# Attention scores as 64x64 tiles in the four quarters of the array, with two PSUM banks fewer for turned rows and probabilities

## The reference, cut to what matters

```python
# q, k, v: (4, 8, 576, 64);  window 128
scores = q @ k.T / 8                       # per batch and head
mask = (rel >= 0) & (rel < 128)            # rel = query position - key position
scores = where(mask, scores - slope[head] * abs(rel), -1e9)
attn = softmax(scores);  x = attn @ v      # x: 2304 rows of 512
x = moe(x, w_gate, w1, w2)                 # each token to one of 8 experts, 288 tokens each, by sorted logits
h = x @ w_in;  out = (h * sigmoid(h)) @ w_out
```

## Time and profile before

| | |
|---|---|
| time, 3 runs | 860.46, 860.61 (median), 862.47 us |
| the profiled execution: its time, its span | 861.91 us, 860.2 us |
| busy share of the span: PE, PEld, DVE, ACT, POOL | 96%, 90%, 57%, 38%, 36% |
| scores in attention, 192 columns | 224 matmul records |
| DMA queues, share of 16 engines | 28.7% for the main queue over the span |

### The profile page before, as it was taken

One profiled execution on the slowest core, in us unless ns is written; L12 is line 12 of the kernel. 1 busy time (PEld: TensorE's weight loads), 2 busy tenths in 40 slices (PEclk: granted clock), 3 DMA queues, 4 the chain that ended last, 5 costly groups with the idle time before them and its releaser, 6 DMA issues.

```text
span 860.2 us, 17129 instructions
## 1 busy us (share of the span) xinstructions
PE 827.4 (96%) x6459; PEld 773.0 (90%) x6459; DVE 494.5 (57%) x1590; ACT 330.3 (38%) x767; POOL 306.7 (36%) x336
## 2 busy tenths in 40 slices
PE   5999999937999999999999999999999999999997
PEld 5999999926988998999899888998998899899996
DVE  7778787665855666475655443756556566542111
ACT  3655566513323432433343224333432433343221
POOL 1443333502435323523433235234332623433223
PEclk9999999957999999999999999999999999999999
DMA  9887888305104303230430040404301240431000
GB/s 148 179 169 160 174 165 172 103 14 171 54 1 126 111 13 98 67 86 2 126 106 18 1 126 13 123 2 126 99 26 45 83 123 2 127 88 36 1 1 37
DMA packets 154626, 71.39 MB, mean 83 GB/s; under 512 B 98992, under 2 KB 140976, under 8 KB 154544
## 3 DMA queue, kind: packets, MB, share of 16 engines
q1 hardware_dynamic: 149200, 60.56, 28.7%
q0 software_dynamic: 2976, 9.44, 3.6%
q10 hardware_dynamic: 2368, 0.30, 0.3%
HBM read 60.83 MB, written 9.44 MB: 82 GB/s over the span
## 4 chain that ended last, share of the span: by engine, by line
PE 74%; DVE 3%; POOL 1%; issue 1%; DMA 1%; ACT 0%; SPq 0%; POOLq 0%; DVEq 0%
PE hp L1127 12%; PE hp L1128 11%; PE hp L1129 11%; PE acc L1212 8%; PE acc L1214 8%; PE acc L1213 8%; PE acc L1127 4%; PE acc L1129 4%; PE acc L1128 4%; PE rt L1079 2%; DVE test L1379 1%; DMA wa_raw<-in_moe_w_dram 1%; PE rt L1094 0%; DVE test L1375 0%; PE acc L1121 0%
## 5 line engine op out<-in xcount | busy, mean ns | idle before, releaser
L1055 POOL TENSOR_TENSOR h_l<-h_raw,h_h 128x256 fp32r<-128x256 f32 (+1 forms) x128 | 115.5, 903 | 265.5 <-ACT h_h L1336 265.3
L1605 DVE TENSOR_TENSOR h_raw<-hp,gate 128x256 f32<-128x256 f32 (+1 forms) x128 | 58.5, 457 | 179.9 <-ACT gate L1328 179.0
L1127 PE MATMUL hp<-xy_h,res_h 128*128 128x256 f32 (+1 forms) x512 | 154.0, 301 | 0.0
L1128 PE MATMUL hp<-xy_l,res_h 128*128 128x256 f32 (+1 forms) x512 | 151.4, 296 | 0.0
L1129 PE MATMUL hp<-xy_h,res_l 128*128 128x256 f32 (+1 forms) x512 | 151.2, 295 | 0.0
L1043 POOL TENSOR_TENSOR wb_l<-wb_raw,wb_h 128x512 fp32r<-128x512 f32 x64 | 86.6, 1354 | 125.6 <-ACT wb_h L1272 125.5
L1328 ACT ACTIVATE gate<-hp 128x256 f32<-128x256 f32 (+1 forms) x128 | 52.6, 411 | 195.4 <-PE hp L1129 193.7
L1212 PE MATMUL acc<-res_h,h_h 128*128 128x512 f32 x288 | 116.7, 405 | 0.0
L1214 PE MATMUL acc<-res_h,h_l 128*128 128x512 f32 x288 | 113.5, 394 | 0.0
L1213 PE MATMUL acc<-res_l,h_h 128*128 128x512 f32 x288 | 113.5, 394 | 0.0
L1127 PEld LDWEIGHTS hp<-xy_h,res_h 128*128 128x128 f32 x512 | 96.5, 188 | 3.6
(11 more groups left out here) (216 smaller groups left out, 1684.3 us busy)
## 6 DMA issues: line engine op xcount, KB each, us to landing
wa_raw<-in_moe_w_dram SPq DMA_DIRECT2D x64, 256.0 KB, 3.3
wb_raw<-in_moe_w_dram SPq DMA_DIRECT2D x64, 256.0 KB, 3.0
k_rows<-in_k_dram SPq DMA_DIRECT2D x64, 72.0 KB, 3.7
q_rows<-in_q_dram SPq DMA_DIRECT2D x60, 72.0 KB, 2.7
v_rows<-in_v_dram SPq DMA_DIRECT2D x32, 128.0 KB, 2.5
stage<-in_moe_w_in_dram SPq DMA_DIRECT2D x8, 512.0 KB, 4.6
x_rows<-x_rows_sb SPq DMA_DIRECT2D x16, 256.0 KB, 4.2
stage<-in_moe_w_out_dram SPq DMA_DIRECT2D x8, 512.0 KB, 4.3
```

The costliest lines, as they stand in the source:

```text
L1055: pool.tensor_tensor(h_l[:, cols], h_raw[:, cols], h_h[:, cols].bitcast(FP32), ALU.subtract).then_inc(g_low, 1)
L1127: nc.tensor.matmul(out_, weights_h, cols_h, start=start, stop=False)
L1128: nc.tensor.matmul(out_, weights_h, cols_l, start=False, stop=False)
L1605: nc.vector.tensor_tensor(h_raw[:, h_cols(s, f)], hp[(A_NO[s, f] - 1) % 2][:, 0:width], gate[:, 0:width], ALU.mult).then_inc(g_done, 1)
```

## The change

Scores are computed without the zero blocks. For each unit and each head there is one matmul with 64 rows and 64 columns of weights, placed with `tile_position` in one quarter of the array. Head 0 uses rows 0 to 63, head 1 rows 64 to 127. An even unit's heads go to columns 0 and 64, an odd unit's to 64 and 0, so that two units with two heads name each quarter once. Even and odd units have banks of their own (`s_even`, `s_odd`, two each). In odd units head 1 therefore stands on partitions 0 to 63: `bias` has a form for each parity, and `turn_probs` writes their two heads in reverse. `t_ps` and `m_ps` have one bank each. `turn_probs(s)` now waits for `copy_probs(s - 1)`. The end of the turned output rows comes a slot later than the main part, `gate_logits` two slots later than `turn_x_main`, and `add_logits` a slot later than before.

```diff
 def unit_col(u):
     return {0: KEYS, 1: KEYS + U, UNITS - 1: 0}.get(u, KEYS * (u % 2))
+def bank_col(u):
+    return KEYS if u == 0 else 0
...
-        qT = [sb(f"qT{i}", [P, UNITS, P]) for i in range(2)]
+        qT = [sb(f"qT{i}", [P, S]) for i in range(2)]
...
-        s_ps, t_ps, o_ps, m_ps = pb("s_ps"), pb("t_ps"), pb("o_ps"), pb("m_ps")
+        s_ps = [pb("s_even"), pb("s_odd")]
+        t_ps, o_ps, m_ps = pb("t_ps", 1)[0], pb("o_ps"), pb("m_ps", 1)[0]
+        x_banks = [(m_ps, m_ps)] * (NG - 1) + [(s_ps[0][1], s_ps[1][1])]
...
             def turn_x_main(g):
-                if g >= 1:
-                    pe.wait_ge(x_taken, g)
+                if 1 <= g < NG - 1:
+                    pe.wait_ge(lg_added, g)
...
             def turn_x_end(g):
-                if g >= 1:
-                    pe.wait_ge(lg_added, g)
+                pe.wait_ge(x_taken, g + 1)
...
             def scores(s):
                     k0, kw = unit_keys(u)
-                    c = unit_col(u)
-                    last = nc.tensor.matmul(s_ps[s % 2][:, c:c + kw], qT[g % 2][:, u, :], kT[g % 2][:, k0:k0 + kw],
-                                            start=True, stop=True)
+                    c = bank_col(u)
+                    for h in range(2):
+                        at, side = slice(U * h, U * (h + 1)), h ^ (u % 2)
+                        to = slice(U * side, U * (side + 1))
+                        last = nc.tensor.matmul(s_ps[u % 2][s % 2][to, c:c + kw], qT[g % 2][at, U * u:U * (u + 1)],
+                                                kT[g % 2][at, k0:k0 + kw], start=True, stop=True,
+                                                tile_position=(U * h, U * side))
                 last.then_inc(s_done, 1)
...
             def turn_probs(s):
                 pe.wait_ge(exp_done, UNITS_TO[s + 1])
-                if s >= 2:
-                    pe.wait_ge(pT_ready, s - 1)
+                if s >= 1:
+                    pe.wait_ge(pT_ready, s)
...
                 if kind == 2 and g >= 1:
                     turn_x_main(g - 1)
+                if kind == 3 and g >= 1:
                     turn_x_end(g - 1)
-                if kind == 3 and g >= 1:
-                    gate_logits(g - 1, slice(0, TB))
+                if kind == 0 and g >= 2:
+                    gate_logits(g - 2, slice(0, TB))
             turn_x_main(NG - 1)
             weighted_values(NS - 1)
-            pe.wait_ge(lg_added, NG - 1)
             gate_logits(NG - 1, slice(0, main_tiles(NG - 1)))
...
                 if kind == 3 and g >= 1:
                     copy_x(g - 1)
-                    copy_x_end(g - 1)
+                if kind == 0 and g >= 2:
+                    copy_x_end(g - 2)
                 if s + 1 < NS:
                     exponentials(s + 1)
                 copy_probs(s)
...
-            def turn_q(g, h):
+            def turn_q(g):
...
-                nc.vector.transpose(qT[g % 2][at, :, at],
-                                    q_rows[g % RING_IN][at].rearrange("p n d -> p (n d)").rearrange("p (u m) -> p u m", m=U)
-                                    ).then_inc(q_turned, 1)
+                nc.vector.transpose(qT[g % 2][:], q_rows[g % RING_IN][:].rearrange("p n d -> p (n d)")).then_inc(q_turned, 1)
...
+            def make_bias(pair):
+
+                nc.vector.scalar_tensor_tensor(bias[:, pair], steep[:], 2.0 ** (-16.0 * pair / H),
+                                               masked[:, None, :].to_broadcast([P, 2, KEYS]), ALU.mult, ALU.add
+                                               ).then_inc(bias_ready, 1)
```

More of the change, by code:

```diff
@@ L454, in turn_probs @@
                     region, parity = divmod(n, 2)
-                    to = t_ps[s % 2][:, 2 * P * region:2 * P * (region + 1)].rearrange("p (h u m) -> p h u m", h=2, u=2)
-                    last = nc.tensor.transpose(to[:, :, parity, :], from_, ident[:])
+                    to = t_ps[:, 2 * P * region:2 * P * (region + 1)].rearrange("p (h u m) -> p h u m", h=2, u=2)
+                    to = to[:, ::-1 if parity and (s % 4 or region) else 1, parity, :]
+                    last = nc.tensor.transpose(to, from_, ident[:])
                 last.then_inc(t_done, 1)
@@ L548, in copy_probs @@
                 w = slice(2 * P if s == 0 else 0, 2 * P if s == NS - 1 else 4 * P)
-                nc.scalar.activation(pT[s % 2][:, w], t_ps[s % 2][:, w], ACT.Copy).then_inc(pT_ready, 1)
+                nc.scalar.activation(pT[s % 2][:, w], t_ps[:, w], ACT.Copy).then_inc(pT_ready, 1)
             load_squares(act, q_rows, q, 0, q_loaded[0])
@@ L675, in _ @@
             nc.vector.memset(p_first[:, U:P], 0.0).then_inc(pads_ready, 1)
[L676 to L681, removed]
+            for side in range(2):
+                dve.wait_ge(pool_seq, 1)
+                at = slice(U * side, U * (side + 1))
+                for parity in range(2):
+                    nc.vector.tensor_scalar(steep[at, parity, :], rel[at, :], -float(U) * side,
+                                            -(D ** 0.5) * 2.0 ** (-8.0 * ((side ^ parity) + 1) / H), ALU.add, ALU.mult
+                                            ).then_inc(steep_ready, 1)
             nc.vector.tensor_scalar(rel[U:P, :], rel[U:P, :], -float(U), None, ALU.add).then_inc(rel_ready, 1)
@@ L691, in _ @@
             dve.wait_ge(dve_seq, 3)
[L692 to L695, removed]
+            dve.wait_ge(steep_ready, 4)
+            def make_bias(pair):
+                nc.vector.scalar_tensor_tensor(bias[:, pair], steep[:], 2.0 ** (-16.0 * pair / H),
+                                               masked[:, None, :].to_broadcast([P, 2, KEYS]), ALU.mult, ALU.add
+                                               ).then_inc(bias_ready, 1)
+            make_bias(0)
             turn_k(0)
-            turn_q(0, 0)
-            turn_q(0, 1)
-            dve.wait_ge(bias_ready, PAIRS)
+            turn_q(0)
+            dve.wait_ge(bias_ready, 1)
             bias_and_max(0)
@@ L702, in _ @@
             bias_and_max(1)
-            turn_q(1, 0)
+            turn_q(1)
             for s in range(NS):
                 g, kind = divmod(s, 4)
-                if kind == 0 and g >= 2:
+                if kind == 1 and g >= 2:
                     add_logits(g - 2)
                 if s + 2 < NS:
+                    if kind == 2 and 1 <= g + 1 < PAIRS:
+                        dve.wait_ge(bias_ready, g + 2)
                     bias_and_max(s + 2)
+                if kind == 0 and g + 1 < PAIRS:
+                    make_bias(g + 1)
                 if s >= 1:
@@ L714, in _ @@
                 if kind == 3 and g + 2 < NG:
-                    turn_q(g + 2, 0)
-                if kind == 0 and g + 1 < NG:
-                    turn_q(g + 1, 1)
+                    turn_q(g + 2)
                 if kind >= 1 and g >= PAIRS + 1 and g % PAIRS == 1:
                     rank_batch(g // PAIRS - 1, kind - 1)
+            add_logits(NG - 2)
             normalise(NS - 1)
```

35 lines of the change are left out of this document (15 added, 20 removed).

## The result

The changed kernel took 867.47 us (median of 4 runs, 866.88 to 868.99) against 860.6 us (4 runs, 860.46 to 862.47): a ratio of 1.0075, 95% interval 1.0062 to 1.0087, slower by 6.9 us. The forecast was 888 us. The sign came out as forecast and the size did not. The experiments show that the sign was luck: the scores themselves became faster, and these four executions were slower for another reason. Of twelve more executions of the same kernel, half were faster than the kernel before (experiment 9).

A forecast was written before the change was run, and what follows sets the result against it. PE was taken to bound steady attention, so only its queue counted. +27.0 us for scores and +0.5 for the end, on the median 860.6, gave 888 us; range 845 to 908, likeliest case 876 to 900.

The forecast's parts named there:

- (a): Scores' arithmetic: quarters start in order, eight records filling five periods, 0.815 us a plain slot, 0.16 us more than before.
- The weight loads, as a bound: Lower bound of a slot's scores: eight weight loads following each other at 0.054 us, 0.43 us.
- (b): Change between full array and quarters, twice a slot: 0.33 us a slot, the upper end, taken as a choice.
- The sum of the scores: Plain slot's scores, arithmetic plus mode changes: 1.145 us, 0.44 more than 0.70; +27.0 us over 16 pairs.
- overlap in full, and border in full: Rival for slot scores: 0.43 + 0.33 = 0.76 us against 0.70, no change within a few us, 858 to 867; chance 0.10.
- starts in order, borders free: Rival for slot scores: ordered starts cost 8.6 us, mode changes nothing; 869 us, spread 864 to 874; chance 0.17.
- (c): `turn_q`, one transpose of 128 partitions for two of 64: DVE saves 0.77 us a pair, time gains nothing.
- (d): Probabilities' one bank: `turn_probs(s)` waits for `copy_probs(s - 1)`, with 0.74 us of cover; taken as nothing.
- (e): Output rows in one bank, chain stretched one step a slot: nothing, at worst 0.3 us a pair (5 us).
- (f): End of attention: last pair but one's gate matmuls a slot later, one wait gone; within 1 us, +0.5 in the sum.
- (g): Start: first scores a microsecond or two earlier, gain given back at pair 1's queries and slot 2's maximum; nothing.
- a third way: Way the forecast could be wrong, to the slow side: granted clock below 1.00 in steady attention; no size given.

The follow-up runs named there:

- experiment 9: Changed kernel without an edit, twelve more executions: six from 858.27 to 859.14 us, six from 866.64 to 884.57 us; ratio 1.0014.
- experiment 12: Changed kernel with five filling transposes, each slot's score matmuls issued twice from slot 8 on: 878.14 us in one execution.
- experiment 7: Changed kernel with five filling transposes, odd units' heads not in reverse, so four matmuls share two quarters: 875.13 us in one execution.
- experiment 8: Kernel before, full-width scores, with only the change's single banks and later output rows, gate and addition: 861.72 us against 861.53, 1.0007.
- experiment 1: Kernel before with 40 transposes of the identity ahead of its first scores: 861.19 us against 861.52, 0.9996.
- experiment 4: Changed kernel with five transposes of the identity in PE's pause at 11 us: 857.79 us against 861.52, 0.9955.
- experiment 5: Changed kernel with three matmuls in one quarter filling the pause at 11 us: 867.52 to 875.72 us, 1.0106.
- experiment 11: Changed kernel with five transposes of the identity in slot 1, where PE does not wait: 859.29 us against 861.69, 0.9967.
- experiment 13: Changed kernel with three matmuls in one quarter added in slot 1: 868.69 to 886.03 us, median 874.3, 1.0143.
- experiment 14: Changed kernel with five transposes in the pause at 11 us, timed again: 858.49 us against 861.45, 0.9958.
- experiment 6: Changed kernel with 16 transposes of the identity in slot 4: 860.69 us against 861.53, 1.0008.
- experiment 10: Changed kernel with 38 transposes ahead of the scores and 18 in the pause behind the first turned probabilities: 858.32 us against 861.69, 0.9956.
- experiment 2: Changed kernel with 38 transposes of the identity ahead of its first scores: 867.18, 867.46, 875.04 and 884.53 us.
- experiment 3: Kernel before, slot 3's scores made to wait for slot 2's maxima, so PE pauses: 863.02 us against 861.52, 1.0017.

## Why the prediction was wrong

**(a) failed.** "The next quarter's first record can start beside it but not ahead of it" is the step, "it" being a quarter's second record. All four first records started within 0.02 us of each other, 0.2 us ahead of any second one, and the four quarters then ran together: 0.33 us for the block and not 0.815 (experiment 12). The matmuls keep their order, but in each of the two rounds by itself. The 0.163 us between a quarter's own records was right once the block was running (0.21 us in the first round), and experiment 7 shows where it binds: two matmuls that share a quarter follow each other.

**The weight loads, as a bound, failed too.** I gave the full overlap at least eight times 0.054 us, 0.43. All eight start within 0.07 us (84.50 to 84.57), those of one round within 0.02 us, and the rounds follow each other at the 0.163 us of streaming, so the loads bind nothing. Matmuls in different quarters start as close together. The Trainium skill, "TensorE: Matmul & The Clock Gate", Part 3, has matmuls in different tiles start about 4 ns apart; the rows have the first records of all four within 0.02 us, so the trace agrees with it.

**(b) held.** 0.33 us a slot was forecast for the two borders, as a choice of the upper end, and 0.30 measured: 0.14 on the way in (0.09 and 0.05) and 0.16 on the way out (0.10 and 0.06). The borders cost nearly as much as the whole block. The Trainium skill, "TensorEngine Tiling (Array Packing)", Tiling Modes, has a change of mode drain TensorE; the trace agrees in that each change has a price, though it does not show that the array is empty.

**The sum of the scores** is then 0.33 + 0.30 = 0.63 us a plain slot against 0.70, -0.07 and not +0.44; over 16 pairs of 0.24 us about -4 us and not +27. The rival "overlap in full, and border in full" (chance 0.10) had the mechanism. It gave 0.76 us because of the wrong bound for the block. The time of 867.47 us lies in the band of another rival, "starts in order, borders free" (864 to 874), but neither half of that one is right. In the chances, half of 0.10 was entered as 0.06 and not 0.05; nothing hangs on it.

**(c), (d), (e) held.** DVE is busy 13.3 instead of 15.7 of 20 us and PE as full as before, so its saving bought nothing to be seen, and neither experiment 8 nor the changed kernel shows a wait of PE in steady attention. **(f)** was mis-sized: at most 1 us was given to the end, 1.4 us it is (experiment 8), though 1.1 of it only moves there from the start, which I had overlooked. **(g)** was put at nothing. The first scores start at 8.31 and not 9.13 us, and slot 8 starts 1.9 us sooner in the early execution of experiment 9, of which 1.1 us are the gate matmuls that moved. That transfers and maxima bound the start is borne out by experiment 1 for the kernel before.

**The clock was named but not priced.** I wrote that a fall of the granted clock in steady attention would be a third way. None came there. What came was a later rise at the start, in 10 of 16 executions, which the sum had at nothing. It is worth 9.5 us between the two executions with traces, and it alone turns a kernel of 858.5 us into one of 867 or more, so that the forecast "slower" came true by luck. That added full-array work makes the rise early, and added quarter work does not, is shown by experiments 4, 5, 11, 13 and 14 together. Why one execution without an edit rises at 15.7 us and another at 36.7 is open: the instructions are the same.

**The tail**, from slot 60 to the first matmul behind attention, goes by where the clock falls. The gate matmuls that moved account for 1.4 of the 3.5 us (17.7 us in experiment 8). With quarter-size scores it is also 17.7 us where the clock fell behind attention's last matmul (experiment 6). It is 18.2 us where the clock fell ahead of the last gate matmuls (171.1 us, experiment 11), 18.4 where it fell ahead of the last output rows (169.3 us, experiment 9), and 19.6 and 19.8 where it fell ahead of the last values (experiment 14 and the result). What decides the moment of the fall was not tried.

The five transposes of experiment 4, repeated in experiment 14, are the version to keep: 0.9955 and 0.9958 of the kernel before, 3.7 and 3.0 us less, and no late execution in 9. The longer filling of experiment 10 does no better (0.9956, none of 6 late).

## What to carry to other kernels

Packing four 64x64 matmuls beside each other works for fp32 at full value (four in the time of one full-width matmul), provided that each quarter is named once in a round. But price the borders with the full array first, here 0.30 us for every 0.33 us of block, and put as much quarter work between two borders as banks allow. A change that makes TensorE's work lighter can cost more in the clock than it saves in matmuls, here in the first 37 us: look at the length of a known record, such as a transpose, from the start to the first rise, and not at the column of the granted clock alone. Time such a kernel often enough to see both heaps. The first four executions here were all late and said slower; of the next twelve, half were 3 us faster than the kernel before.

## What the runs showed of the hardware that was not expected

PE can be full for 24 us and stay at 1.2 GHz: from 12.0 to 36.7 us of the changed kernel it never paused, and its mix of quarter-size scores, transposes and short value matmuls did not bring the rise in this execution. With five more transposes of the identity (1.2 us) near the start, all 15 executions were early, and so were all 6 with 18 in the pause (experiment 10). With six quarter-size records in the place of the five, none of ten was.

A clock raised before the kernel's real work does not stay up by itself: in experiment 2 it fell at 12.2 us, at the end of a pause of 1.88 us, and came back only at 36.1 us. In experiment 3 a pause of 0.69 us did not lower it.

Head 0 and head 1 of a unit, on different rows of the array, write into one PSUM bank on different partitions, and their records start together (`s_even` x2 at 84.50 us) without slowing each other.
